# Three preparation steps re-ordered in a fused attention, soft-MoE and top-2-MoE kernel: who zeroes and loads the halo, when VectorE scales the slot weights, and where the expert weights land

## The reference

```python
# 1. causal 7-tap convolution, one softmaxed tap vector per head (8 heads)
w = softmax(weight)                      # 8 x 7
y[b, s] = sum_k w[head, k] * x[b, s - 6 + k]
# 2. soft MoE, 8 experts with 4 slots each
logits = y @ phi                         # N x 32
d = exp(logits - logits.max(0)); d /= d.sum(0)
slot_input = d.T @ y                     # 32 x 192
slot_out[e] = relu(slot_input[e] @ w1[e]) @ w2[e]     # 192 -> 1024 -> 192
z = softmax(logits, axis=1) @ slot_out   # N x 192
# 3. noisy top-2 MoE, 8 experts
noisy = z @ w_gate + log1p(exp(z @ w_noise)) * noise
out[i] = sum over the two best experts of gate * (relu(z[i] @ v1[e]) @ v2[e])
```

## Time and profile before

| | |
|---|---|
| median of 3 runs | 944.5 us (943.0 to 944.6) |
| the profiled execution: its time, its span | 943.0 us, 941.2 us |
| PE busy | 881.7 us (94%) |
| DVE busy | 637.3 us (68%) |
| ACT busy | 460.3 us (49%) |
| POOL busy | 346.3 us (37%) |
| HBM read, written | 63.41 MB, 27.77 MB |

### The profile page before, as it was taken

How to read it: one execution, slowest core, us unless ns; L and a number is a source line. 1 busy time by engine, 2 the same in 40 slices (tenths; PEclk the granted TensorE clock), 3 DMA queues, 4 the chain that set the end, 5 groups by cost and what they waited for, 6 DMA issues and landing times. The chain is left out here.

```text
span 941.2 us, 25954 instructions
## 1 busy us (share of the span) xinstructions
PE 881.7 (94%) x7807; PEld 712.7 (76%) x7808; DVE 637.3 (68%) x1520; ACT 460.3 (49%) x961; POOL 346.3 (37%) x384
## 2 busy tenths in 40 slices
PE   5999989999786979999999999999999999999995
PEld 4999988996453447888777777777777777777773
DVE  4133245467479959888777777777777777777773
ACT  2222221223141645555666666666666666666662
POOL 5000000001001033333346666556666566666552
PEclk9999999999765979999999999999999999999998
DMA  8366898999987022333344444444444444444441
GB/s 246 114 191 212 248 321 260 320 332 258 280 224 229 0 73 81 91 88 88 102 113 110 113 113 110 107 115 112 110 114 106 113 109 114 111 112 106 117 114 25
DMA packets 93722, 138.89 MB, mean 148 GB/s; under 512 B 10764, under 2 KB 63356, under 8 KB 91752
## 3 DMA queue, kind: packets, MB, share of 16 engines
q1 hardware_dynamic: 75100, 120.49, 43.3%
q0 software_dynamic: 17536, 16.91, 10.8%
q10 hardware_dynamic: 1036, 0.81, 0.4%
HBM read 63.41 MB, written 27.77 MB: 97 GB/s over the span
## 5 line engine op out<-in xcount | busy, mean ns | idle before, releaser
L1611 PE MATMUL ps<-w2hl,x_ring 128*128 x1848 | 339.4, 327 | 0.0
L1262 DVE SCALAR_TENSOR_TENSOR x_ring<-ps,x_ring 128x512 f16<-128x512 f32 x462 | 297.1, 685 | 17.3 <-ACT x_ring L753 14.0
L753 ACT ACTIVATE x_ring<-ps 128x512 f16<-128x512 f32 x462 | 250.7, 594 | 107.7 <-PE ps L1590 105.0
L1611 PEld LDWEIGHTS ps<-w2hl,x_ring 128*128 128x128 f16 x1848 | 171.4, 98 | 90.6 <-issue 1.0
L598 POOL DMA_INDIRECT stage<-pay_rows,row_id x146 | 142.6, 976 | 256.0 <-PE ps L1590 189.8
L609 POOL DMA_INDIRECT out_rows<-x_ring,row_id x146 | 182.5, 1250 | 58.3 <-issue 42.5
L1615 PE MATMUL ps<-w2hl,x_ring 128*128 x1848 | 190.8, 246 | 1.0 <-DVE x_ring L1262 1.0
L1615 PEld LDWEIGHTS ps<-w2hl,x_ring 128*128 128x128 f16 x1848 | 160.0, 98 | 31.4 <-DVE x_ring L1262 1.4
L1590 PE MATMUL ps<-c,x_ring 96*128 96x128 f16 x1848 | 142.4, 220 | 0.5 <-DVE c L1255 0.5
L1590 PEld LDWEIGHTS ps<-c,x_ring 96*128 96x128 f16 x1848 | 120.6, 98 | 0.8 <-issue 0.7
L759 ACT ACTIVATE x_ring<-ps,scl 128x192 f32<-128x192 f32 x146 | 61.5, 421 | 116.1 <-PE ps L1615 116.1
(11 more groups left out here) (329 smaller groups left out, 714.8 us busy)
## 6 DMA issues: line engine op xcount, KB each, us to landing
x_ring<-a_room SPq DMA_DIRECT2D x231, 192.0 KB
x_ring<-in_x SPq DMA_DIRECT2D x14, 1536.0 KB, 7.1
stage<-in_moe_w SPq DMA_DIRECT2D x24, 768.0 KB, 11.3
out_rows<-zero SPq DMA_DIRECT2D x14, 768.0 KB, 10.3
a_room<-in_moe_w SPq DMA_DIRECT2D x13, 768.0 KB, 11.1
gate_room<-in_moe_w SPq DMA_DIRECT2D x8, 768.0 KB, 11.9
stage<-pay_rows,row_id POOLq DMA_INDIRECT x146, 2.8
out_rows<-x_ring,row_id POOLq DMA_INDIRECT x146, 2.4
```

The source lines that it names most:

```text
L753: a.activation(hh[:, m % 2, 4 * half:4 * half + 4, :].rearrange("p j q -> p (j q)"), ps[:, 2 + 2 * (m % 2) + half, :], ACT.Relu).then_inc( ...
L1262: last = v.scalar_tensor_tensor(hl[:, m % 2, 4 * half:4 * half + 4, :].rearrange("p j q -> p (j q)"), ps[:, 2 + 2 * (m % 2) + half, :], 0. ...
L1611: t_.matmul(ps[:, 6 + b % 2, 0:2 * D], hh[:, m % 2, j, :], w, start=k == 0 and j == 0, stop=False)
```

## The change

Seven edits, all ahead of the blocks:

1. `x_halo` is zeroed whole by POOL, as its first instruction (128 x 1152 fp32), instead of four rows by DVE. SP waits for it, then issues all eight halo loads, and only then the x chunks. ACT issues none.
2. ACT issues the loads of gate weights and noise ahead of the exponential of the taps.
3. DVE forms the tap table in four waited steps instead of three, two of them waited, and `phi_r` in 14 instructions of 96 x 32 instead of 7 of 96 x 64.
4. `h_t` is zeroed by POOL, behind the sum over partitions and `g_ps`, instead of by ACT.
5. On DVE the last three `c_scale` stand ahead of the wait for `csum_all`, mixed with the last two `low_half`, instead of behind the slot input.
6. The seventh and eighth slot w1 go to `gate_room` and wait for the second pair instead of the first; slot w2 4 and 5 go to `stage1`; 6 and 7 go to the rooms of slot w2 0 and 1 in `stage2`, each when that expert's matmuls are done (so_ps 1 and 2). All four slot w2 0 to 3 are issued ahead of `load_late(1)`.
7. The `again` loads have new rooms and waits (so_ps 4, 6, 8), and the four writes of zeros stand ahead of the last two of them.

```diff
-        again_rooms = [stage2[:, 0:2 * F], a3_room[:, :].bitcast(F32)[:, 0:2 * F],
-                       a3_room[:, :].bitcast(F32)[:, 2 * F:4 * F], stage1[:, 0:2 * F], stage1[:, 2 * F:4 * F],
+        again_rooms = [a3_room[:, :].bitcast(F32)[:, 0:2 * F], a3_room[:, :].bitcast(F32)[:, 2 * F:4 * F],
+                       stage1[:, 0:2 * F], stage1[:, 2 * F:4 * F], stage2[:, 0:2 * F],
...
-            if e < WR:
-                return w2s[e], w2s_in[e], 16 * (2 * E // WR + 1)
-            if e < WR + 2:
-                return w2_late[e - WR], w1s_in[e - WR + 2], 16 * (E // WR + 2)
-            return w2_late[e - WR], w1_late_in[e - WR - 2], 48
+            if WR <= e < WR + 2:
+                return w2_late[e - WR], w2_late_in[e - WR], 16
+            at = e if e < WR else e - WR - 2
+            return w2s[at], w2s_in[at], 16 * (2 * E // WR + 1 + (1 if e >= WR else 0))
...
+            sp.wait_ge(halo_zero, 1)
             runs = S // T
-            for b in range(B // 2):
+            for b in range(B):
...
             load_late(0)
-            for n in range(2):
+            for n in range(WR):
                 load_w2(2 * E + n, s_w2_v)
             sp.wait_ge(x_used, 2 * NCH)
             sp.wait_ge(d_sum, NCH)
             load_late(1)
-            load_w2(2 * E + 2, s_w2_v)
-            sp.wait_ge(w1s_used, E + 2)
-            for i in range(2):
-                sp.dma_start(w1s(E + WR + 2 + i), s_w1_v[WR + 2 + i]).then_inc(w1s_in[i], 16)
-            load_w2(2 * E + 3, s_w2_v)
+            for n in range(WR + 2, E):
+                load_w1(E + n, s_w1_v)
             for e in range(WR, E):
-                if e == WR:
-                    sp.wait_ge(w1s_used, E + 4)
-                elif e == WR + 2:
-                    sp.wait_ge(w1s_used, 2 * E)
+                if e >= WR + 2:
+                    sp.wait_ge(so_ps, e - WR - 1)
...
                 if e == 0:
-                    sp.wait_ge(so_ps, 2)
-                elif e == 1:
                     sp.wait_ge(so_ps, WR)
-                elif e == 3:
+                elif e == 2:
+                    sp.wait_ge(so_ps, WR + 2)
+                elif e == 4:
                     sp.wait_ge(so_ps, E)
                 elif e == 5:
                     sp.wait_ge(cg_ready, 1)
                 elif e == 6:
+                    for k in range(NCH + 4, T // 8 + 1):
+                        zero_out(k)
                     sp.wait_ge(a_ps, 2)
                 sp.dma_start(w1_again(e), t_w1_v[e]).then_inc(again_in[e % 6], 16)
-            for k in range(NCH + 4, T // 8 + 1):
-                zero_out(k)
...
             g = nc.gpsimd
+            g.memset(x_halo[:, :, :], 0.0).then_inc(halo_zero, 1)
...
+            pool.wait_ge(g_ps, 1)
+            g.memset(h_t[:, :, :], 0.0).then_inc(slots_zero, 1)
...
-            for b in range(B // 2, B):
-                lo = b * runs
-                mid = lo + runs // 2
-                act.dma_start(x_halo[lo + 1:mid + 1, :, :], x_v[lo:mid, T - PAD:T, :]).then_inc(halo_in, 16)
-                act.dma_start(x_halo[mid + 1:lo + runs, :, :],
-                              x_v[mid:lo + runs - 1, T - PAD:T, :]).then_inc(halo_in, 16)
-            act.wait_ge(w_cent, 1)
-            a.activation(w_all[:, :, :], w_all[:, :, :], ACT.Exp).then_inc(w_exp, 1)
...
             act.dma_start(noise_s[:, :, :], noise_v).then_inc(noise_in, 16)
+            act.wait_ge(w_cent, 1)
+            a.activation(w_all[:, :, :], w_all[:, :, :], ACT.Exp).then_inc(w_exp, 1)
...
-            act.wait_ge(consts, 1)
-            act.wait_ge(g_ps, 1)
-            a.activation(h_t[:, :, :], zero16[:, 0:1].unsqueeze(2).to_broadcast([P, FJ, E * (NS + SL)]), ACT.Copy
-                         ).then_inc(h_zero, 1)
...
-            for b in range(B):
-                first_row = b * (S // T)
-                v.memset(x_halo[first_row:first_row + 1, :, :], 0.0).then_inc(halo_zero, 1)
...
             for dt in range(TAPS):
-                last = v.tensor_tensor(phi_r[:, :, dt, :], phi_s[:, :, :],
-                                       w_t[:, :, PAD - dt:PAD - dt + 1].to_broadcast([DC, 2, NS]), ALU.mult)
+                for c in range(2):
+                    last = v.tensor_scalar(phi_r[:, c, dt, :], phi_s[:, c, :], w_t[:, c, PAD - dt:PAD - dt + 1],
+                                           None, ALU.mult)
...
-            low_half(NCH - 1)
             c_centre(NCH - 1)
-            low_half(NCH)
+            c_scale(NCH - 3)
+            for e in range(NCH - 1, E):
+                low_half(e)
+                c_scale(e - 1)
             dve.wait_ge(csum_all, 1)
...
-            for b in range(NCH - 3, NCH):
-                c_scale(b)
             step(v.memset(gate_bd[:, :, :], 0.0))
```

26 lines of the change are left out of this document (10 added, 16 removed).

## The result

The changed kernel takes 960.8 us (957.7 to 961.0, four runs) where the kernel before takes 944.4: ratio 1.0174, interval 1.0156 to 1.0191, 16.4 us slower. The prediction was 956.2 us, range 951.0 to 960.0: the direction and most of the size were right, the time lies 0.8 us above the range.

A forecast was written before the change was run, and what follows sets the result against it. With the blocks unchanged, it took the middle as a chain of PE and DVE waits, decided by SP's load queue. Middle +14.5 and start -2.8 gave +11.7 us, profiled 943.0 to 954.7, median 956.2 us; range 951.0 to 960.0.

The forecast's parts named there:

- the twelve instructions: DVE ahead of g_w: the three c_scale moved there make PE's slot input 5.5 us later.
- The eighth slot w1: Middle: issued after pair 2, it lands 8.2 us after the first issue, at 247.9 instead of 239.9; sum so far +8.0.
- Pair 4: PE's fourth slot w1 pair, after its load wait: stays at 3.64 us, at half clock.
- the queue's sum: SP's loads from expert 0's end to the last slot_matrices pair: 39.0 us, making that pair +14.5 us; the queue decides.
- The start: Kernel start: halo loads on SP let PE start earlier, and the gain reaches 224 us whole: -2.8 us (+1.8 to -4.0).
- h_t on POOL: Ahead of g_w: POOL's memset beside DVE's c_scale and low_half costs 0, with up to 2.3 us kept for the range.
- Pairs 1 and 2: First slot w1 pairs after PE's idle gap: half clock, 7.3 us instead of 5.3, +1.9 us (0 if clock holds).
- Slot w2 6 and 7: Middle: number 6 waits for expert 0 and takes 4.6 us, number 7 lands 2.4 later; +1.9 us for PE.
- A: Rival: the zeros ahead of the last again loads delay nothing, so the PE and DVE chain decides: 951.6 us; chance 0.13.
- B: Rival: the clock holds through PE's gap ahead of g_w, all following 2.3 us earlier: 953.9 us; chance 0.12.
- C: Rival: the start gives 0 to +1.8 through late x chunk, noise load or slow memset: 959 to 960.8 us; chance 0.10.
- D: Rival: not slower, as moved gaps let PE keep full clock through the middle; at best 944 us; chance 0.03.

The follow-up runs named there:

- e1: Changed kernel with the four writes of zeros put back behind the last two again loads: 956.9 us, ratio 1.0149.
- e8: Kernel before with the start's edits, and one late slot w2 load moved behind the seventh and eighth slot w1: 944.2 us, ratio 1.0005.
- e17: Kernel before with the start's edits and 28 unused PE transposes ahead of the second pass: 941.9 us, ratio 0.9976.
- e18: Kernel before with the start's edits and unused PE transposes, 13 ahead of the second pass and 11 ahead of pair 4, second measurement: 940.5 us, ratio 0.9956.
- e4: Kernel before with the start's edits alone (halo loads on SP, ACT's loads moved ahead, table in fourteen instructions): 942.5 us, ratio 0.9989.
- e14: Changed kernel with 28 unused PE transposes in the 3.93 us gap ahead of the second pass: 964.9 us, ratio 1.0172.
- e11: The changed kernel itself, measured again on another chip: 967.1 us, ratio 1.0191.
- e12: Changed kernel with h_t zeroed by ACT again, measured beside e11: 965.4 us, ratio 1.0170.
- e3: Changed kernel with h_t zeroed by ACT again, first measurement: 960.5 us, ratio 1.0177.
- e13: Changed kernel with 60 unused PE transposes in the gap ahead of g_w: 964.5 us, ratio 1.0164.
- e5: Changed kernel with the first five again loads waiting for all eight slot experts: 961.4 us, ratio 1.0188.
- e16: Changed kernel with h_t on ACT and unused PE transposes, 28 ahead of the second pass and 50 ahead of g_w: 960.6 us, ratio 1.0117.
- e7: Kernel before with only the four writes of zeros moved ahead of the last two again loads: 948.4 us, ratio 1.0051.

## Why the prediction was right, and where it missed

The direction and the chain were right; three terms of the sum were mis-sized, and they all erred to the same side.

**What held.** g_w decides when PE gets its slot input, and the twelve instructions cost 5.5 us: from the sum over chunks to g_w it was 5.85 us before and is 12.78 now, 6.93 more, of which 1.5 are the collision. The eighth slot w1 landed 8.7 us after the seventh was issued, summed as 8.2. Pair 4 stayed at 3.64 us. The queue decides at the last pair, and PE waits there for a DMA: 4.7 us, where I had said some 8. The rates behind the queue's sum were right: 3.2 us for each again load (five landings at 270.0, 273.2, 276.4, 279.6 and 282.6; the sixth came 1.9 us later), 7.4 for the zeros (7.1), 5.7 for the last two (5.5). The blocks are unchanged in every profile of the chips of e1 to e8, e17 and e18 (600 us).

**Where 5.3 us were missing.** The last pair was summed to 292.4 and came at 297.73. Step by step:

| step | summed | measured | missed by |
|---|---|---|---|
| start, as seen at DVE's sum over chunks | -2.8 | -1.1 | +1.7 |
| sum over chunks to g_w | +5.5 | +6.9 | +1.4 |
| from g_w to the end of expert 0 | 25.8 | 25.5 | -0.3 |
| end of expert 0 to the last pair | 39.0 | 41.5 | +2.5 |

*The start.* The step that failed is "the first two passes are bound by PE, so the gain reaches 224 us whole". The gain was 2.7 us at 140 us although PE started only 1.9 us earlier, since the first pass won some more on the way: its second chunk was through at 34.9 against 37.5. Behind it the half clock that follows the gap of 3.93 us ended at the same moment in both kernels and took 1.6 us back. How much it takes differs from one execution to the next, since the half clock there lasted from some 3 to 6 us; the 1.6 us are those of this pair of profiles. e4 measured 1.0 us for the whole start, and e14 gives 1.8 us more when that gap is filled. That the gap of the earlier trace rows was followed by half clock I had used in the middle, and had not looked for the same pattern at 140 us. The other miss in this step was the landing, 4.6 us instead of 3.2. It has the sign of the rule that I had cited from the Trainium skill, DMA: Bandwidth & Descriptors, section "Issuing engines are not separate DMA queues", that transfers interleave whichever engine starts them; the measured gain of 1.9 us at PE's start nonetheless stands on the other side of the +1.8 that this rule alone would have given.

*h_t on POOL.* "I take 0" was wrong on DVE: g_w came 1.5 us later by it in the profile. What that costs in the time is not settled, 2.0 us less without it between e11 and e12 and nothing in e3. Two instructions ran beside the memset. The tensor_reduce kept its 0.68 us; the tensor_scalar on 16 numbers suffered, and that is just the kind that the page SBUF — State Buffer of the Trainium skill, section "Who interferes with whom", names for a POOL instruction that only writes. The trace agrees. I had cited the rule and weighed it by the size of the instruction; what counts is the length of the memset that it has to sit out, 2.02 us, less what had already run.

*Pairs 1 and 2.* The term (+1.9) came out as +0.7 for the pairs (6.1 us against 5.3), since full clock returned in the middle of pair 2; but the short matmuls ahead of them ran at half clock too and took 0.6 us more. e13 prices the whole gap at 2.5 us, with an error of 2.

*Slot w2 6 and 7, and the queue.* Number 6 took 4.7 us (4.6 summed). Number 7 landed 5.9 us behind it, not 2.4. It was handed over 1.6 us later, since expert 1 has to be through, and the first again loads, handed over at 259.9, then shared the engines with it. e5 shows the sharing: without them 3.5 us. The price of 2.4 came from the earlier trace rows, a pair with nothing handed over behind it until 249.7. Number 7 and the six again loads took 23.6 us together where I had 21.6; that is 2.0 of the 2.5 us. It is a mis-sized term, and the mechanism stands. e5 also shows that the order within this sum is free: number 7 sooner, again loads later, same end.

*Closure.* With the collision taken away and both gaps filled (e16) the ratio is 1.0117, which is 11.0 us of 944.4. The sum of the prediction without its +1.9 for half clock was 9.8 us, and 2.5 for the queue make it 12.3. So the causes together account for the miss to about 1.3 us, within the interval of that run. How it is divided among them rests on single profiles and on differences at the edge of the error.

**The rivals.** A is refuted by e7, where the zeros cost 4.8 us, and e1 agrees (2.4 us, and 3.6 at the last pair). Its argument that completion overlaps failed against one rate for each kind of transfer. B did not act: the clock fell. Its 2.3 us came near to e13's 2.5 by luck. C, "start gives nothing or costs", came closest in its number, 959 to 960.8, and partly for its reason: the start gave 1.0 to 1.1 instead of 2.8, but not through its x chunk or its memset, and the rest of the miss came from the collision and the queue. D did not appear: the middle's clock fell from 0.75 to 0.67, as waits were moved and none removed. The range missed by 0.8 us because it took the bounds of the start, the collision and the queue one at a time, and all three fell on the slow side together. Its upper end, 960.0, also cut through the band of rival C, 959 to 960.8, in which the time lies.

## What to carry to other kernels

A wait of PE is also a matter of clock: read the granted clock behind every gap of PE, at all places and not only where the change is, and price a gain ahead of such a gap at what is left behind it. Price a step that is moved onto the chain together with what the other engines do in that moment, above all an elementwise instruction of DVE beside a long one of POOL. And sum a queue over all that is in it, at one rate for each kind of transfer; a single load's place in it tells nothing of the end.
